# Experts stage: TensorE's loop over the jobs entered twice, the turns of the first rows inside its body

## The chip, the cores and the metric

One Trainium2 chip, one of its cores. The metric is the device time of one execution in microseconds (us), as the median of several runs; lower is better. All matrices are float32; the kernel splits each operand into a high and a low part and takes three products for one.

## The reference, cut to what matters

```python
x = attention(q, k, v)              # 4 x 12 heads, 448 rows, 64 wide, rms-normed q and k
x = x.reshape(1792, 768)            # N tokens, D wide
idx = argmax(norm(x) @ norm(expert_emb).T / tau, axis=1)      # one of 8 experts for a token
for e in range(8):                  # experts
    mask = idx == e
    h = maximum(x[mask] @ w1[e], 0)             # 768 -> 1024
    out[mask] = gate[mask, None] * (h @ w2[e])  # 1024 -> 768
return (sigmoid(out @ w_gate) * (out @ w_val)) @ w_out        # layer 2: 768 -> 1536 -> 768
```

The change is in the second of the three stages, `experts`.

## The kernel before, in words

**Stages.** `attention` (to about 326 us of the profile) computes the tokens' rows, the expert of each and the sorted order; `experts` runs to about 648 us, `layer2` from there to the end. Each engine has an instruction stream of its own; they meet at semaphores. Between two stages is a barrier of all engines.

**Jobs.** The tokens of an expert are taken in jobs of up to T = 294. A job is described by a column of a small table in SBUF, `c.table`, with five rows of J + 1 entries: first token, expert, whether the job is long (more than TS = 256 tokens), column of the list of token numbers, and the number of jobs. VectorE computes it at the start of the stage (`job_table`, L1472 to L1497) and tells by `table_ready`. Each engine reads what it needs from the table into registers of its sequencer with `value_load` (`jobs` at L1286, `long_job` at L1274 and others); in the profile such a load is a TENSOR_LOAD, a FUSED_REGOPS and a SEQ_ASSERT of the helper's line, behind a FUSED_REGOPS for the address when the index is a register. Here there are 8 jobs, 6 short and 2 long.

**One job on TensorE** (`job`, L1592): eight blocks of the first layer (`h`, L1578), each 6 x 3 matmuls, then six blocks of the second (`y`, L1585), each 8 x 3 matmuls, and between the latter the turns (transposes, L1563) of the next job's rows, 6 x 3. Every matmul has a weight load. In the stream the body of a job stands twice, for 256 columns and for 294 (L1625 to L1630): the loop over the jobs (`pe.Fori(0, n_jobs)`) loads `is_long`, and runs the short body or jumps over it (L1627), then jumps over the long body or runs it (L1629), then jumps back (L1625). TensorE's sequencer issues instructions to the array ahead of their execution.

**The start of the stage on TensorE** (L1607 to L1624): 36 idle turns on `tx[0]` (`keep_busy`, L1602), the number of jobs from the table, a wait for cleared banks and for the copied list of tokens, two turns of that list (`tokens_turned`, L1612), six idle turns, a wait for `tokens_out`, and then three times four idle turns and six turns of the first rows (L1621), as each third of the rows has been loaded and scaled by its gates (`gated_dve`, `gated_act`). Then comes the loop.

**The other engines at that point.** GpSimd issues the loads of the first rows (`fetch_rows`, L1110) and then waits in its own loop for turned rows and the first product. ScalarE copies slots of layer 2's weights, scales the second third of the rows (L1436), and takes the high parts of the turned rows (L1422). VectorE, in this order: job table, clearing of banks (L1501), low part of the first weights (`w1_split`, L1457), one slot, wait for `tokens_turned` and copy of the turned list (L1511), scaling of the first third (L1532), `w1_split`, scaling of the last third, two slots, the low parts of the turned rows (L1520), four slots, then its loop (L1548). SP writes the list when it is copied and loads the weights of job 0 once the rows are turned (L1316 to L1319).

**Constants.** GpSimd writes 19 small constants in the fourth step of attention (`constants`, L152), each with a wait for the one before.

Of the kernel before, what the change touches and what calls it, by code (L numbers as in the profile page):

```python
# [145 lines left out]
    return r  # L146


CONSTS = 19


def constants(nc, c, r, pool):  # L152

    done = [0]

    def const(i):
        i.then_inc(r.consts, 1)
        done[0] += 1
        pool.wait_ge(r.consts, done[0])
    exact = dict(allow_small_or_imprecise_dtypes=True)  # L160
    J = MAXJOBS
    const(nc.gpsimd.iota(r.rank[:, :, :], [[0, EARLY], [-1, E]], base=E, channel_multiplier=0, **exact))
    const(nc.gpsimd.iota(r.cap[:, :], [[LINES * CHUNKS, E]], base=0, channel_multiplier=0, **exact))
    const(nc.gpsimd.memset(r.half[:, :], 0.5))
    const(nc.gpsimd.memset(r.ones[:, :], 1.0))
    const(nc.gpsimd.memset(r.tri[:, :], 1.0))
    const(nc.gpsimd.affine_select(out=r.tri[:, :], in_=r.tri[:, :], compare_op=ALU.is_ge, fill=0.0, base=0,
                                  pattern=[[-1, P]], channel_multiplier=1))
    const(nc.gpsimd.memset(c.ones8[:, :], 1.0))
    const(nc.gpsimd.memset(r.mask_e[:, :, :], 1.0))  # L170
    const(nc.gpsimd.memset(r.mask_e[:, :, 0], 0.0))
    const(nc.gpsimd.memset(r.mask_l[:, :, :], 1.0))
    const(nc.gpsimd.memset(r.mask_l[:, :, 0], 0.0))
    const(nc.gpsimd.iota(r.lines[:, :], [[1, ROWS]], base=0, channel_multiplier=0, **exact))
    const(nc.gpsimd.iota(r.slots[:, :], [[1, SLOTS]], base=0, channel_multiplier=0, **exact))
    const(nc.gpsimd.iota(r.token[:, :].rearrange("p (b t) -> p b t", t=NT), [[S, B], [1, NT]], base=0,
                         channel_multiplier=NT, **exact))
    const(nc.gpsimd.iota(c.thr[:, :, :], [[0, E], [T, NT + 3]], base=0, channel_multiplier=0, **exact))
    const(nc.gpsimd.memset(c.thr[:, :, 0], -1.0))
    const(nc.gpsimd.iota(c.jnum[:, :, :], [[1, J + 1], [0, E]], base=0, channel_multiplier=0, **exact))  # L180
    const(nc.gpsimd.iota(c.vals[:, 1, :], [[1, E]], base=0, channel_multiplier=0, **exact))
    const(nc.gpsimd.iota(c.vals[:, 3, :], [[CHUNKS, E]], base=0, channel_multiplier=0, **exact))
    assert done[0] == CONSTS


# [1038 lines left out]
def experts(nc, c, w1, w2, w_l2, w_sums, x_rows, table_of_slots, ids):  # L1224
# [4 lines left out]
    with ExitStack() as ctx:  # L1229
# [17 lines left out]
        index_in = sem("index_in")  # L1247
        dve_table = sem("dve_table")
        table_ready = sem("table_ready")
        tokens_turned = sem("tokens_turned")  # L1250
        tokens_out = sem("tokens_out")
        slots_written = sem("slots_written")
# [21 lines left out]
        def long_job(eng, j):  # L1274
            return eng.value_load(c.table[0:1, bass.ds(j + 2 * (J + 1), 1)], min_val=0, max_val=1)
# [175 lines left out]
        def _(dve):  # L1451
# [20 lines left out]
            def job_table():  # L1472
# [23 lines left out]
                chain(nc.vector.tensor_scalar(c.tablef[:, 2, :], c.tablef[:, 2, :], float(TS), None, ALU.is_gt))  # L1496
                nc.vector.tensor_copy(c.table[:, :], c.tablef[:, :, :].rearrange("p a j -> p (a j)")).then_inc(table_ready, 1)  # L1497

            job_table()
            for bank in hb + yb:  # L1500
                nc.vector.memset(bank[:, TS:T], 0.0).then_inc(banks_set, 1)  # L1501
# [43 lines left out]
                x_out(0, kd, first_banks[kd])  # L1545
            for k in range(3, 7):
                slot_low(k)
            with dve.Fori(0, n_jobs) as j:  # L1548
                job_order(w1_split, w2_split, h_out, scale, x_out, lambda j, d: None, j)

        @block.tensor
        def _(pe):
# [51 lines left out]
                for _ in range(turns):  # L1604
                    nc.tensor.transpose(bank[:, 0:128], c.ident[:, :], c.ident[:, :])

            keep_busy(tx[0], 36)  # L1607
            n_jobs = jobs(pe, pe.wait_ge)
            pe.wait_ge(banks_set, HB + YB)
            pe.wait_ge(tokens_copied, 1)  # L1610
            for part in range(2):
                nc.tensor.transpose(hb[2][0:HALF, part * 128:part * 128 + LINES],  # L1612
                                    c.tokens[0:LINES, part * HALF:(part + 1) * HALF],
                                    c.ident[0:LINES, 0:LINES]).then_inc(tokens_turned, 1)
            keep_busy(hb[0], 6)
            pe.wait_ge(tokens_out, 1)
            for a in range(GATHERS):
                keep_busy(hb[0], 4)
                pe.wait_ge((gated_dve, gated_act)[a % 2], a // 2 + 1)
                for kd in range(KD):  # L1620
                    last = nc.tensor.transpose(first_banks[kd][:, a * R:(a + 1) * R], xr[0:R, a, kd * 128:(kd + 1) * 128],  # L1621
                                               c.ident[0:R, 0:R])
                    if a == GATHERS - 1:
                        last.then_inc(x_turned, 1)  # L1624
            with pe.Fori(0, n_jobs) as j:  # L1625
                is_long = long_job(pe, j)
                with pe.If(is_long < 1):  # L1627
                    job(j, TS)
                with pe.If(is_long > 0):  # L1629
                    job(j, T)  # L1630


def layer2(nc, c, w_l2, w_sums, ids_dram, out):
# [435 lines left out]
def build(nc, q, k, v, g_q, g_k, emb, tau, w1, w2, w_gate, w_val, w_out, out):  # L2069
# [4 lines left out]
    with ExitStack() as ctx:  # L2074
# [12 lines left out]
        with ExitStack() as kept:  # L2087
            def far(name, shape, dt=F32):
                return kept.enter_context(nc.sbuf_tensor(name, shape, dt, side="right"))
            c.table = far("table", [1, 5 * (MAXJOBS + 1)], I32)  # L2090
            c.raw1 = far("raw1", [128, 4, KD, 128])
            c.W1H = far("W1H", [128, 2, KD, 128], F32R)
            c.W1L = far("W1L", [128, 2, KD, 128], F32R)
# [70 lines left out]
```

## Time and profile before

| | |
|---|---|
| Median of 3 runs | 1143.29 us (1142.89 to 1144.02) |
| The profiled execution | 1147.7 us, its span 1146.2 us |
| Mean granted clock of TensorE | 0.986 |
| PE busy | 1110.0 us (97%), 7378 matmuls and turns |
| PEld (weight loads) busy | 983.0 us (86%), 7379 |
| DVE busy | 776.2 us (68%) |
| ACT busy | 600.0 us (52%) |
| POOL busy | 367.7 us (32%) |

Times in the profile are microseconds from the start of the span. PE is TensorE's array, PEld its weight loads; a q behind an engine's name (PEldq) marks an instruction of its sequencer, which keeps no array busy: branches, register operations, loads from SBUF into registers, waits. A group's row reads: line, engine, operation, tiles written and read, shape, count | busy us, mean ns of one | idle us before them, and what ended the idle time; "issue" means that no other engine's signal did. The granted clock is the share of full speed that TensorE had.

### The profile page before, as it was taken

How to read it: one execution, taken by the hardware profiler on the slowest of the kernel's cores; microseconds unless marked ns; L12 is line 12 of the kernel's file. 1: busy time of each engine (PE TensorE's matmuls, PEld its weight loads, DVE VectorE, ACT ScalarE, POOL GpSimd, SP SyncE). 2: the span in 40 equal slices, each digit the busy share in tenths (PEclk: the TensorE clock that was granted, in tenths of full speed). 3: DMA queues.
4: the chain of work that ended last, by engine and by line, in shares of the span. 5: the costliest groups of instructions: out<-in, count | busy, mean ns of one | idle time of the engine just before them, and what ended most of it. 6: DMA issues, size and time to landing. Idle time of an engine off the chain costs nothing. (4 is left out here: it accounts for less than half of the span.)

```text
span 1146.2 us, 22052 instructions
## 1 busy us (share of the span) xinstructions
PE 1110.0 (97%) x7378; PEld 983.0 (86%) x7379; DVE 776.2 (68%) x1411; ACT 600.0 (52%) x1415; POOL 367.7 (32%) x367
## 2 busy tenths in 40 slices
PE   7999999999979899999999899999999999999997
PEld 6666666666679899999999899999999999999997
DVE  5778888897776455665556886475569675574672
ACT  4877877877536455565555653242245343441441
POOL 7797888888531110111011502000003012000002
PEclk9999999999989899999999999999999999999999
DMA  4345564543438666786688342242331334331312
GB/s 125 92 138 164 167 202 144 151 119 109 126 76 210 165 179 172 210 213 187 168 207 220 96 125 83 63 125 63 97 111 42 111 106 151 102 104 49 112 42 97
DMA packets 207778, 149.62 MB, mean 131 GB/s; under 512 B 12446, under 2 KB 203550, under 8 KB 207718
## 3 DMA queue, kind: packets, MB, share of 16 engines
q1 hardware_dynamic: 203446, 133.79, 41.9%
q0 software_dynamic: 3568, 14.82, 4.4%
q8 instruction: 35, 0.57, 0.2%
q10 hardware_dynamic: 704, 0.23, 0.1%
q14 instruction: 25, 0.20, 0.1%
HBM read 128.29 MB, written 20.53 MB: 130 GB/s over the span
## 5 line engine op out<-in xcount | busy, mean ns | idle before, releaser
L2027 PE MATMUL qb<-BH,l_WH 128*128 128x448 f32 x504 | 185.9, 369 | 3.2 <-DVE BL L1897 3.2
L2029 PE MATMUL qb<-BH,l_WL 128*128 128x448 f32 x504 | 185.9, 369 | 0.0
L2028 PE MATMUL qb<-BL,l_WH 128*128 128x448 f32 x504 | 185.9, 369 | 0.0
L1732 ACT ACTIVATE l_WH<-stream 128x384 fp32r<-128x384 f32 x209 | 100.7, 515 | 127.4 <-PE ob L2050 102.4
L1968 POOL TENSOR_TENSOR quads<-quads 128x448 f32<-128x448 f32 x24 | 30.6, 1277 | 381.8 <-DVE quads L1836 381.8
L1836 DVE TENSOR_TENSOR quads<-qb,quads 128x448 f32<-128x448 f32 x168 | 100.2, 621 | 67.5 <-PE qb L2029 67.3
L1832 DVE TENSOR_TENSOR l_WL<-stream,l_WH 128x384 fp32r<-128x384 f32 x209 | 121.5, 600 | 20.4 <-ACT l_WH L1732 20.4
L803 ACT ACTIVATE PR<-sc,negmax 112x448 f32<-112x448 f32 x192 | 120.7, 641 | 15.5 <-DVE negmax L535 14.7
L1573 PE MATMUL hb<-XH,W1H 128*128 128x256 f32 (+1 forms) x384 | 112.6, 293 | 5.3 <-issue 4.3
L1573 PE MATMUL yb<-HH,W2H 128*128 128x256 f32 (+1 forms) x384 | 112.9, 294 | 0.4 <-DVE W2L L1515 0.4
L2048 PE MATMUL ob<-l_WH,GH 128*128 128x384 f32 x336 | 112.5, 335 | 0.4 <-DVE Y L1916 0.4
L2050 PE MATMUL ob<-l_WH,GL 128*128 128x384 f32 x336 | 112.3, 334 | 0.0
L2049 PE MATMUL ob<-l_WL,GH 128*128 128x384 f32 x336 | 112.3, 334 | 0.0
L1575 PE MATMUL hb<-XH,W1L 128*128 128x256 f32 (+1 forms) x384 | 111.5, 290 | 0.0
L1574 PE MATMUL hb<-XL,W1H 128*128 128x256 f32 (+1 forms) x384 | 111.4, 290 | 0.0
L1574 PE MATMUL yb<-HL,W2H 128*128 128x256 f32 (+1 forms) x384 | 109.8, 286 | 0.0
L1575 PE MATMUL yb<-HH,W2L 128*128 128x256 f32 (+1 forms) x384 | 109.7, 286 | 0.0
L535 DVE TENSOR_REDUCE negmax<-sc 112x2 f32<-112x896 f32 x96 | 101.8, 1083 | 10.5 <-PE sc L928 10.4
L2027 PEld LDWEIGHTS qb<-BH,l_WH 128*128 128x128 f32 x504 | 95.1, 189 | 12.6 <-issue 3.3
L2029 PEld LDWEIGHTS qb<-BH,l_WL 128*128 128x128 f32 x504 | 95.1, 189 | 9.2
L2028 PEld LDWEIGHTS qb<-BL,l_WH 128*128 128x128 f32 x504 | 95.0, 189 | 9.1
L1457 DVE TENSOR_TENSOR W1L<-raw,W1H 128x384 fp32r<-128x384 f32 x132 | 68.1, 557 | 50.4 <-ACT W1H L1411 49.0
(259 smaller groups left out, 2552.5 us busy)
## 6 DMA issues: line engine op xcount, KB each, us to landing
raw<-in_moe_w_dram SPq DMA_DIRECT2D x68, 384.0 KB, 5.2
stream<-in_moe_w_dram SPq DMA_DIRECT2D x48, 512.0 KB, 4.7
stream<-w_sums SPq DMA_DIRECT2D x92, 192.0 KB, 2.4
w_sums<-Sb SPq DMA_DIRECT2D x12, 768.0 KB, 6.3
stream<-in_moe_w_out_dram SPq DMA_DIRECT2D x48, 192.0 KB, 2.4
stream<-in_moe_w_val_dram SPq DMA_DIRECT2D x36, 192.0 KB, 2.8
stream<-in_moe_w_gate_dram SPq DMA_DIRECT2D x33, 192.0 KB, 2.6
raw<-in_q_dram SPq DMA_DIRECT2D x24, 224.0 KB, 3.3
```

Source lines behind the costliest of these rows:

```text
L535: nc.vector.tensor_reduce(negmax[:, n % 2, j, :], sc[j % 2][0:P, :, 0:S], AX.X, ALU.max, negate=True).then_inc(maxed, 1)
L803: nc.scalar.activation(PR[:, h, j, :], sc[j % 2][0:P, h, 0:S], ACT.Exp, bias=negmax[:, s, j, h:h + 1], accum_out=den[:, s, h, j:j + 1]).th ...
L1573: nc.tensor.matmul(out[:, 0:n], WH[:, slot, k, :], mh, start=(k == 0), stop=False)
L1574: nc.tensor.matmul(out[:, 0:n], WH[:, slot, k, :], ml, start=False, stop=False)
L1575: last = nc.tensor.matmul(out[:, 0:n], WL[:, slot, k, :], mh, start=False, stop=(k == blocks - 1))
L1832: nc.vector.tensor_tensor(W(c.WL, n), c.stream[:, n % RING, :], W(c.WH, n).bitcast(F32), ALU.subtract).then_inc(c.w_lo, 1)
L2027: nc.tensor.matmul(bank, wh, bh, start=(k == 0), stop=False)
L2028: nc.tensor.matmul(bank, wh, bl, start=False, stop=False)
L2029: mm = nc.tensor.matmul(bank, wl, bh, start=False, stop=(k == 2))
L2048: nc.tensor.matmul(bank, GH[:, f, at], W(c.WH, slot), start=(f == 0), stop=False)
L2049: nc.tensor.matmul(bank, GH[:, f, at], W(c.WL, slot), start=False, stop=False)
L2050: mm = nc.tensor.matmul(bank, GL[:, f, at], W(c.WH, slot), start=False, stop=(f == 3))
```

## The change

TensorE's loop over the jobs becomes a loop with two passes (`entry` 0 and 1) around a loop over jobs. How many jobs a pass has, and the first one's number, come from four integers in SBUF, `c.entries`. For the first pass they are constants, written by GpSimd: first 0, count 1. For the second VectorE computes them from the table: the first job is 1 if job 0 is short and 0 if it is long, the count is the number of jobs less that. VectorE tells by `entries_known`, once before the job table and once before its own loop. The order in the body is turned round: the long body comes first and only in the second pass, then, only in the first pass, the turns of the first rows (`first_turns`, with 8 idle turns instead of 36 at its head), then a second load of `is_long` and the short body. In the first pass the one job is run if it is short; if it is long, that pass runs the turns alone.

```diff
@@ constants
-CONSTS = 19
+CONSTS = 21
+    const(nc.gpsimd.memset(c.entries[:, 0:1], 0))
+    const(nc.gpsimd.memset(c.entries[:, 2:3], 1))
@@ experts, VectorE
+            dve.sem_inc(entries_known, 1)
             job_table()
...
             for k in range(3, 7):
                 slot_low(k)
+            chain(nc.vector.tensor_scalar(c.late[:, 0, 0:1], c.tablef[:, 2, 0:1], -1.0, 1.0, ALU.mult, ALU.add))
+            only(nc.vector.tensor_copy(c.entries[:, 1:2], c.late[:, 0, 0:1]))
+            nc.vector.tensor_tensor(c.entries[:, 3:4], c.tablef[:, 4, 0:1], c.late[:, 0, 0:1], ALU.subtract).then_inc(dve_table, 1)
+            dve.wait_ge(dve_table, n_dve[0] + 1)
+            dve.sem_inc(entries_known, 1)
             with dve.Fori(0, n_jobs) as j:
@@ experts, TensorE
-            keep_busy(tx[0], 36)
-            n_jobs = jobs(pe, pe.wait_ge)
-            pe.wait_ge(banks_set, HB + YB)
-            pe.wait_ge(tokens_copied, 1)
...
-            with pe.Fori(0, n_jobs) as j:
-                is_long = long_job(pe, j)
-                with pe.If(is_long < 1):
-                    job(j, TS)
-                with pe.If(is_long > 0):
-                    job(j, T)
+            def first_turns():
+
+                keep_busy(tx[0], 8)
+                pe.wait_ge(banks_set, HB + YB)
+                pe.wait_ge(tokens_copied, 1)
...
+
+            with pe.Fori(0, 2) as entry:
+                pe.wait_ge(entries_known, entry + 1)
+                first = pe.value_load(c.entries[0:1, bass.ds(entry, 1)], min_val=0, max_val=1)
+                count = pe.value_load(c.entries[0:1, bass.ds(entry + 2, 1)], min_val=1, max_val=J)
+                with pe.Fori(0, count) as k:
+                    j = k + first
+                    with pe.If(entry > 0):
+                        is_long = long_job(pe, j)
+                        with pe.If(is_long > 0):
+                            job(j, T)
+                    with pe.If(entry < 1):
+                        first_turns()
+                        pe.wait_ge(table_ready, 1)
+                    is_long = long_job(pe, j)
+                    with pe.If(is_long < 1):
+                        job(j, TS)
@@ build
+            c.entries = far("entries", [1, 4], I32)
```

What is left out inside `first_turns` is unchanged: the turns of the list of tokens, the idle turns, and the turns of the first rows with their waits.

## Rows read from the trace of the kernel before

**Rows 1.** The page, busy us and share of the span.

```profile
PE 1110.0 (97%) x7378; PEld 983.0 (86%) x7379; DVE 776.2 (68%) x1411; ACT 600.0 (52%) x1415; POOL 367.7 (32%) x367
```

**Rows 2.** Groups by line and shape, TensorE, 338 to 650 us.

```profile
L1573 PE MATMUL hb<-XH,W1H 128*128 128x256 f32 x288 | 83.6, 290 | 5.3 <-issue 4.3 <-DVE XL L1520 0.6 <-DVE W1L L1457 0.4
...
L1563 PE MATMUL tx<-ident,xr 98*128 98x98 f32 x144 | 18.8, 247 | 0.8 <-DVE XL L1520 0.8
```

**Rows 3.** Timeline of TensorE: start, duration in us, what [idle before it].

```profile
380.79 0.58 PE L1573 MATMUL hb<-XH,W1H 128*128 128x256 f32 x1 [4.34 <-issue]
```

**Rows 4.** Line L1629: count, ns min/median/max, first and last start.

```profile
L1629 PEldq COMPARE_BRANCH  x8: 73/210/4879, 374.2 to 645.7; - x8
```

**Rows 5.** DMA queues in 376:378, 382:650, 650:1146 and 369.8:371.8: packets, MB, share.

```profile
q8 instruction: 1, 0.02, 3.0%
...
q1 hardware_dynamic: 84197, 42.76, 60.8%
q0 software_dynamic: 1904, 7.24, 10.4%
...
q8 instruction: 21, 0.34, 0.3%
...
q8 instruction: 1, 0.02, 4.2%
```

**Rows 6.** Windows: us, PE, PEld, DVE, ACT, POOL busy (count), clock, DMA share, GB/s.

```profile
379.25:386.08 6.83, 5.29 (x25) 5.29 (x26) 0.40 (x1) 0.96 (x3) 0.28 (x1) 0.50 0.21 62
386.08:389.50 3.42, 3.42 (x30) 3.42 (x30) 2.24 (x6) 2.05 (x5) 2.25 (x3) 1.00 0.42 123
...
652.30:655.70 3.40, 3.40 (x11) 2.99 (x10) 3.40 (x8) 3.40 (x8) 0.00 (x0) 0.50 0.26 9
```

**Rows 7.** Lines L1625 and L1275, TensorE's sequencer in 494 to 497 us.

```profile
L1625 PEldq ALU_OP  x1: 36/36/36, 494.9 to 494.9; - x1
L1625 PEldq COMPARE_BRANCH  x1: 213/213/213, 495.0 to 495.0; - x1
L1625 PEldq FUSED_REGOPS  x1: 59/59/59, 495.2 to 495.2; - x1
...
L1275 PEldq TENSOR_LOAD <-table x1: 300/300/300, 495.4 to 495.4; - x1
L1275 PEldq FUSED_REGOPS  x1: 151/151/151, 495.7 to 495.7; - x1
L1275 PEldq SEQ_ASSERT  x1: 18/18/18, 495.9 to 495.9; - x1
```

**Rows 8.** Timeline of TensorE: first products of jobs 4 and 2, of layer 2.

```profile
496.74 0.28 PE L1573 MATMUL hb<-XH,W1H 128*128 128x256 f32 x1
...
419.36 0.40 PE L1573 MATMUL hb<-XH,W1H 128*128 128x294 f32 x1
...
651.11 0.44 PE L2027 MATMUL qb<-BH,l_WH 128*128 128x448 f32 x1 [3.16 <-DVE BL L1897]
```

**Rows 9.** Timeline of TensorE and VectorE at the start of the stage.

```profile
327.04 4.13 PE L1605 MATMUL tx<-ident 128*128 128x128 f32 x36 [1.14 <-PEq L192]
...
337.28 0.33 PE L1621 MATMUL tx<-ident,xr 98*128 98x98 f32 x2
...
338.53 0.58 PE L1573 MATMUL hb<-XH,W1H 128*128 128x256 f32 x1 [0.58 <-DVE XL L1520]
...
332.30 0.34 DVE L1511 CAST tokens_T<-hb 84x196 uint32<-84x196 f32 x1
...
335.93 0.62 DVE L1532 TENSOR_SCALAR xr<-xr 98x768 f32<-98x768 f32 x1 [1.33 <-DMA xr<-x_rows,index]
```

**Rows 10.** Line L1587, the sequencer's step before a block of the second layer, 367:370.

```profile
L1587 PEldq ALU_OP  x1: 36/36/36, 368.3 to 368.3; - x1
```

**Rows 11.** Timeline of GpSimd's constants, and of TensorE at 77 us.

```profile
69.61 0.10 POOL L179 MEMSET thr<- 1x8 f32 x1
...
77.31 0.60 PE L911 MATMUL tqk<-ident,qkn 112*128 112x112 f32 x4 [1.92 <-POOL qkn L307]
```

More of the change, by code:

```diff
@@ L1249, in experts @@
         table_ready = sem("table_ready")
+        entries_known = sem("entries_known")
         tokens_turned = sem("tokens_turned")
@@ L1605, in keep_busy @@
                     nc.tensor.transpose(bank[:, 0:128], c.ident[:, :], c.ident[:, :])
-            keep_busy(tx[0], 36)
-            n_jobs = jobs(pe, pe.wait_ge)
-            pe.wait_ge(banks_set, HB + YB)
-            pe.wait_ge(tokens_copied, 1)
[L1611 to L1624, printed above, removed]
@@ L1625, in _ @@
-            with pe.Fori(0, n_jobs) as j:
-                is_long = long_job(pe, j)
-                with pe.If(is_long < 1):
-                    job(j, TS)
-                with pe.If(is_long > 0):
-                    job(j, T)
+            def first_turns():
+                keep_busy(tx[0], 8)
+                pe.wait_ge(banks_set, HB + YB)
+                pe.wait_ge(tokens_copied, 1)
+                for part in range(2):
+                    nc.tensor.transpose(hb[2][0:HALF, part * 128:part * 128 + LINES],
+                                        c.tokens[0:LINES, part * HALF:(part + 1) * HALF],
+                                        c.ident[0:LINES, 0:LINES]).then_inc(tokens_turned, 1)
+                keep_busy(hb[0], 6)
+                pe.wait_ge(tokens_out, 1)
+                for a in range(GATHERS):
+                    keep_busy(hb[0], 4)
+                    pe.wait_ge((gated_dve, gated_act)[a % 2], a // 2 + 1)
+                    for kd in range(KD):
+                        last = nc.tensor.transpose(first_banks[kd][:, a * R:(a + 1) * R], xr[0:R, a, kd * 128:(kd + 1) * 128],
+                                                   c.ident[0:R, 0:R])
+                        if a == GATHERS - 1:
+                            last.then_inc(x_turned, 1)
```

## The prediction

> **What bounds the kernel now.** First the page: TensorE is busy for 1110.0 of 1146.2 us [rows 1]. Time that TensorE alone wins or loses goes straight into the span, wherever nothing else is late. Next, the groups of instructions of the experts' stage [rows 2]: of 5.3 us of idle time before the first layer's matmuls, 4.3 are put down to "issue", so to no other engine. The timeline places them before 380.79, where job 1 begins [rows 3]. The branch rows of TensorE's sequencer explain them: L1629, the test that skips the long body, ran eight times, one of them took 4879 ns where the median is 210, and the first began at 374.2 [rows 4], before the array was done: the sequencer runs ahead of it. In the DMA view a packet of queue 8, "instruction", falls into 376 to 378; from 382 to 650 that queue has none [rows 5]. So the first jump over code not yet fetched waited for it, and then the whole loop was held. The stop costs more than its idle time: the granted clock was 0.50, TensorE's lower level, from 379.25 to 386.08, after TensorE had stood idle; 25 matmuls took 5.29 us, where at 1.00 30 take 3.42 [rows 6]. 25 x 0.12 = 3.0, so 2.3 more. Together 4.3 + 2.3 = **6.6 us**, all that the change can win here.
>
> **Between two jobs.** The sequencer's steps at 495 [rows 7]: add 0.036, branch back 0.213, address 0.059, table load 0.300, bounds 0.151 and 0.018. Ahead of them stands L1629, taken, 0.210; a branch not taken is its shortest, 0.073 [rows 4]; behind them come a branch not taken and three register operations (0.04 to 0.06) for the waits of the first product. From the start of the add (494.9) to that of the last bound (495.9) are 1.0 us for 0.76 of durations: some 0.06 between two steps. In all 11 steps, 1.2 + 0.66 = 1.9 us, begun at 494.6. The next job's first matmul starts at 496.74 with no gap [rows 8]. So the lead is about 2.1 us and 1.9 fit in; after a long job's matmuls (294 columns instead of 256) the same number of instructions is 2.4 us.
> The same prices for the new loop. The jobs are short, short, long, short, short, long, short, short (the first long one starts at 419.36 [rows 8]).
> - Short to short: add, branch back, add for j, branch, load (4 steps), two taken branches (over the long body, over the turns), a second load (4), branch, three register operations: 18 steps, 2.05 + 18 x 0.06 = 3.1 us. Less 2.1, and 0.1 because the weight load isn't ahead either: 1.1 idle, twice.
> - Long to short: branch, load, branch first, then the same: 24 steps, 3.0 + 1.4 = 4.4; less 2.4, plus 0.1: 2.1 idle, twice.
> - Short to long: 1.8, hidden as now, twice.
> - Job 0 to job 1, by the outer loop, two loads of entries more: 30 steps, 3.3 + 1.8 = 5.1; less 2.1, plus 0.1: 3.1 idle, but no fetch: what it jumps to has been there.
> Plain boundaries: 2 x 1.1 + 2 x 2.1 = **+6.4 us**.
> The Trainium skill ("Advanced Engine Details and Errata", Control Flow Timing) gives about 108 ns for a compare-and-branch; that lies between the trace's 0.073 for one not taken and 0.21 for one taken. With its figure for the taken ones the plain boundaries would come to about 4.8, an estimate.
>
> **Clock after the new gaps.** 3.4 us at 0.50 lose 1.5 by [rows 6]. The 3.16 us gap before layer 2 [rows 8] was followed by 0.50 from 652.3 to 655.7 [rows 6]. So for the 3.1 us gap +1.5. For the two of 2.1 no row decides: bounds 0 and 3.0, I take the middle, +1.5. For those of 1.1 I take 0.
>
> **The start.** TensorE now comes to its far jump at once: free at 327.0 (its turns start at 327.04 [rows 9]), two loads of entries at 0.8 each, a few register steps: jump at 329.2. It skips the long body, 647 instructions by the code (288 matmuls and 18 turns, each with a weight load, and 35 waits), which are not there. For the stop I take the one measured, 4.88, bounds 3.8 and 4.9 (the packet came late in a busy DMA then): 334.1. What hides it now: 36 idle turns until 331.17 and the rows' turns after them. The cover is too short in two places.
> First, VectorE waits in order for the tokens' turn. It came before its copy at 332.30 [rows 9]; now it comes at 335.4, the copy at 336, the scaling of the first rows, the weight split and then the scaling of the last rows follow at their old distances (0.74, 0.53, 1.0), the last at about 338 instead of 335.93 [rows 9]. With the slack behind it: **+1.6** at least.
> Second, code comes in packets: 21 for layer 2's 5040 matmuls and weight loads and 187 waits, about 250 instructions each [rows 5]. The one in 369.8 to 371.8 [rows 5] is asked for when the sequencer enters new code, some 2 us before (374.2 to 376.6 at the jump). Around 368.3 it issued L1587 of y(4) [rows 10], by the code 542 instructions into the short body, 702 from the start of TensorE's block, give or take 10. The new jump's target is at 667: some 35 instructions before that edge, and the turns have 93. The next packet is asked for on arrival, and takes 1.5 to 2 to start, 1 to transfer and 1.5 until use: about 4.3, so 338.4. Then some 25 turns of 0.112 (4.13 / 36 [rows 9]) are left before the last rows' turns, 2.8, and 1.25 from those to the first product (337.28 to 338.53 [rows 9]): 342.4 instead of 338.53, **+3.9 us**, high end 5.0. The first product is slow already now (0.58 us long [rows 9]) and will be: 0.
>
> **Small items.** GpSimd gets two memsets in its row of constants, 0.10 each [rows 11] and as much for the wait behind each; the work after them is on the way to the product for which TensorE waits 1.92 us at 77.31 [rows 11]: **+0.4**, bounds 0 and 0.4. VectorE's sem_inc and five small operations before its loop, about 0.7, fall into a wait for ScalarE there; without that cover, 0.7. SP's loads of weights and GpSimd's next gather are issued after the turns and the first product as before, and shift along; no queue is passed. TensorE's short waits for VectorE inside jobs (0.4 and 0.8 us [rows 2] and some as short) shrink, since the others catch up in the new gaps: -1.2.
>
> **Sum**: 3.9 + 0.4 - 6.6 + 3.1 + 1.5 + 6.4 + 1.5 - 1.2 = +9.0 us. The profiled execution took 1147.7 (span 1146.2), 4.4 above the median of 1143.29; taken to the median, **1152.3 us**.
>
> **Rivals.**
> 1. The stop is hidden under the rows' load and the boundaries stay hidden. It decides if the sequencer's lead is over 4.4 us, not 2.1. Then the 6.6 goes and 0.4 comes: 1137.1, faster. Against it: L1629 began at 374.2, and the array ran out at 376.45. Chance 0.09.
> 2. One stop at the start only (the target lies past the edge, or two packets come at once) and no slow clock after the 2.1 us gaps: 1.6 + 0.4 - 6.6 + 3.1 + 1.5 + 6.4 - 1.2 = +5.2, or +3.7 if the clock also holds after the 3.1: 1147.0 to 1148.5. Chance 0.16.
> 3. The steps between jobs cost 1 us less than I count (a load or test merged): gaps 2.1, 1.1, 1.1, 0, 0. With the start of rival 2, 1.6 + 0.4 - 6.6 + 2.1 + 2.2 - 1.2 = -1.5: 1141.8; with mine 1144.1. Chance 0.05.
> 4. The loop, some 120 instructions longer, is no longer held, and jumps fetch again: 6.6 at each of six more boundaries, about 1190. The present loop jumps back over 1300 instructions seven times without a packet [rows 5], so chance 0.02. The Trainium skill ("Runtime: NRT & Kernel Launch", Instruction fetch mechanics) says that a taken branch to outside a window of two blocks must fetch; by that rule this rival would be right, and today's loop would stop seven times, which the trace denies.
> The forecast has 0.68.
>
> **Numbers.** 0.2% (2.3 us) is about what a measurement of this kernel can tell from no change. Faster by more: 0.09 (rival 1); within: 0.06 (rival 3 and a tail of 2); slower: 0.85. The range takes in rival 2, half of 3 and nearly all high ends (5.0 for the start, 3.0 for the clock, gaps a tenth longer): 1144.5 to 1158.
>
> **What would show it.** Right: a compare-branch of TensorE of 4 to 5 us at about 329, a second stop of the array until about 338, the first product near 342; no long branch after that; idle time put down to "issue" of about 3.1 us before job 1 and 2.1, 1.1, 2.1, 1.1 before jobs 3, 4, 6, 7. Wrong: jobs that follow without a gap, or a first product at 338.5.

## The result, and the profile after

The changed kernel takes **1152.2 us** (median of 6 runs, 1149.94 to 1155.64); the kernel before, run beside it, 1143.91 (1142.89 to 1147.10). The ratio is 1.0072, 95% interval 1.0052 to 1.0091: slower by 8.3 us, where 9.0 had been forecast. The profiled execution took 1151.0 us, its span 1149.5.

The spans of the two profiled executions differ by 3.3 us only. Attention was 4.3 us shorter in the one of after: TensorE's block of the stage begins at 322.5 instead of 326.8 (the rows of its first signal, below). The profile of before has three spells of the lower clock in attention, 6.8 us at 24.3, 3.4 us at 78.9 and 6.8 us at 317.8; that of after has only the last of them (6.8 us at 313.4). At 1.5 us for 3.4 us of the lower level [rows 6] the two others make some 4.5 us, an estimate. Such spells come and go from run to run in code that nobody touched. So lengths inside the experts' stage are compared here.

The first signal of TensorE's block by its line, in the kernel before and in the one after:

```profile
L1553 PEldq EVENT_SEMAPHORE  x1: 51/51/51, 326.8 to 326.8; - x1
```

```profile
L1562 PEldq EVENT_SEMAPHORE  x1: 51/51/51, 322.5 to 322.5; - x1
```

**The jump.** The branch over the long body in the first pass, by its line, from 322 to 332 us, is a stop of the forecast size (4.88 had been taken):

```profile
L1642 PEldq COMPARE_BRANCH  x1: 4476/4476/4476, 325.0 to 325.0; - x1
```

No other execution of it in the stage is long (median 0.087 us), and from 370 to 652 us queue 8 has no packet of instructions: the new loop is held too.

**The start**, timeline of TensorE:

```profile
329.64 1.96 PE L1614 MATMUL tx<-ident 128*128 128x128 f32 x8 [8.07 <-issue]
331.40 0.53 PE L1622 MATMUL hb<-ident,tokens 98*84 98x98 f32 x2
331.73 2.31 PE L1614 MATMUL hb<-ident 128*128 128x128 f32 x10
...
335.76 0.33 PE L1631 MATMUL tx<-ident,xr 98*128 98x98 f32 x2
...
337.02 0.38 PE L1582 MATMUL hb<-XH,W1H 128*128 128x256 f32 x1 [0.58 <-DVE XL L1524]
```

VectorE's timeline, copy of the turned list and scaling of the first and last thirds:

```profile
331.97 0.36 DVE L1515 CAST tokens_T<-hb 84x196 uint32<-84x196 f32 x1 [3.92 <-PE hb L1622]
332.93 0.62 DVE L1536 TENSOR_SCALAR xr<-xr 98x768 f32<-98x768 f32 x1 [0.60 <-issue]
...
334.40 0.62 DVE L1536 TENSOR_SCALAR xr<-xr 98x768 f32<-98x768 f32 x1
```

Against [rows 9] the copy comes 9.5 us after the stage's first signal instead of 5.5, the last scaling after 11.9 instead of 9.1, the first product after 14.5 instead of 11.7: **+2.8**. The second stop of the array that I had forecast, until about 338, is not there. What is there: 8 idle turns in 1.96 us, twice as long each as the 36 of [rows 9] (4.13). TensorE had stood idle for 8.07 us and got the lower clock. From 329.64 to the last of the rows' turns it has no idle time: 46 turns in a row, 20 of them at the lower clock. VectorE's last scaling is done at 335.02, and the turns that need it begin only at 335.76. So the array's own row of turns set the first product, and VectorE's late list did not.

The 2.8 compares two single profiles. In the profiles of the five kernels below that start as the kernel before does (the one with two more reads, the one with more constants, the three with its hint) the first product comes 10.8 to 12.5 us after the first signal, so against them the changed start is 2.0 to 3.8 us longer.

**The boundaries.** Timeline of TensorE, the first products of jobs 1, 3, 4, 6 and 7; those of jobs 2 and 5 have no idle time ahead:

```profile
377.33 0.38 PE L1582 MATMUL hb<-XH,W1H 128*128 128x256 f32 x1 [2.89 <-issue]
...
458.03 0.38 PE L1582 MATMUL hb<-XH,W1H 128*128 128x256 f32 x1 [1.89 <-issue]
...
495.30 0.39 PE L1582 MATMUL hb<-XH,W1H 128*128 128x256 f32 x1 [0.85 <-issue]
...
574.92 0.38 PE L1582 MATMUL hb<-XH,W1H 128*128 128x256 f32 x1 [1.89 <-issue]
...
613.58 0.38 PE L1582 MATMUL hb<-XH,W1H 128*128 128x256 f32 x1 [0.86 <-issue]
```

The view's idle time leaves out what the last product's modelled end covers. I count a gap from the start of the last product to the start of the next, less the 0.12 us (0.13 behind a long job) between two products. By that count they are 3.05, 0, 2.06, 1.02, 0, 2.06, 1.03; the 4.34 of [rows 3] is 4.50. Forecast: 3.1, 0, 2.1, 1.1, 0, 2.1, 1.1.

**The clock.** Windows of after (columns as in [rows 6]), the turns at the start and then behind the first, the second and the fourth of these gaps:

```profile
329.60:333.90 4.30, 4.26 (x21) 4.25 (x22) 1.33 (x3) 0.94 (x1) 0.00 (x0) 0.50 0.20 51
```

```profile
378.20:381.60 3.40, 3.40 (x18) 3.40 (x18) 0.11 (x1) 0.67 (x2) 0.00 (x0) 0.51 0.08 25
458.00:461.50 3.50, 3.47 (x29) 3.48 (x30) 0.38 (x1) 0.93 (x3) 0.27 (x1) 1.00 0.41 120
576.20:579.60 3.40, 3.40 (x19) 3.40 (x17) 0.82 (x2) 1.24 (x3) 0.48 (x1) 0.50 0.10 30
```

The lower level (0.50) came behind the gap of 3.05 and behind one of the two of 2.06, and kept off behind the other.

**The stage in sum.** From [rows 3, 8, 9] and the rows above, with job 2's first product at 415.00 and layer 2's at 654.39 in after:

| us | before | after | difference |
|---|---|---|---|
| first signal to first product | 11.7 | 14.5 | +2.8 |
| to job 1's first product | 42.26 | 40.31 | -1.95 |
| to job 2's | 38.57 | 37.67 | -0.90 |
| to layer 2's | 231.75 | 239.39 | +7.64 |

Together +7.6, and layer 2 is as long as before (from there to the end 495.1 in both).

### The profile page after: what moved, and what is told of

The parts are those of the page before. It is cut to its first block and busy times, and to the rows that moved or that the text cites. A ratio compares the mean times of both kernels' runs of the same rounds, so it can differ in the third digit from the quotient of the medians.

```text
span 1149.5 us, 22076 instructions
## 1 busy us (share of the span) xinstructions
PE 1103.5 (96%) x7350; PEld 978.5 (85%) x7351; DVE 769.8 (67%) x1414; ACT 599.6 (52%) x1415; POOL 367.2 (32%) x369
## 5 line engine op out<-in xcount | busy, mean ns | idle before, releaser
L537 DVE TENSOR_REDUCE negmax<-sc 112x2 f32<-112x896 f32 x96 | 101.8, 1082 | 11.7 <-PE sc L930 11.6
```

The source lines that it names most:

```text
L537: nc.vector.tensor_reduce(negmax[:, n % 2, j, :], sc[j % 2][0:P, :, 0:S], AX.X, ALU.max, negate=True).then_inc(maxed, 1)
```

## The experiments

"Gaps" are counted as above, for jobs 1 to 7. "Stage" is the time from TensorE's first signal to the start of the last job's last product: 320.9 us in the kernel before, 328.7 in the changed one. Ratios are against the kernel before on the same chip.

### The jump first, the loop left as it was

```diff
+            with pe.Fori(0, 2) as entry:
+                with pe.If(entry > 0):
-            keep_busy(tx[0], 36)
+                    keep_busy(tx[0], 8)
...
+                    with pe.Fori(0, n_jobs) as j:
```

An empty first pass jumps over the turns and the whole loop and back; the loop has its one read and its order.

> The present loop of before (one table load, short body, then long body) is kept whole; a first, empty pass jumps over the turns and the loop to its end and back, and 8 idle turns stand where 36 did. Theory (the stop at the end of job 0 is a first fetch of the code behind the long body, and what makes the change slow is the sequencer's work at the boundaries, not the jump): one long compare-branch of 4 to 5 us about 0.4 us after the stage begins, none later; job 1 follows job 0 within 0.2 us, no boundary gap above 0.2 us; first product 0 to 2 us later than before, counted from the stage's start; in all 4 to 6.5 us faster than before, about 1138.5. Rival (the sequencer does not hold code that it only jumped to; the hold comes from running through it): the 4 to 5 us at the end of job 0 stays, time as before or up to 2 us slower. Rival 2 (the far jump cannot be hidden; the start pays it): first product 4 us later, time within 2 us of before.

Measured: 1145.14 us, ratio 1.0005 (0.9989 to 1.0021). The empty pass stopped 3.75 us at the start (first product after 12.9 us, +1.1, which is less than what such starts differ by). But the stop at the end of job 0 stayed, as the rival has it. The branch over the long body by its line, and the packets of instructions in 372 to 382:

```profile
L1631 PEldq COMPARE_BRANCH  x8: 73/212/4845, 374.3 to 644.9; - x8
```

```profile
q8 instruction: 3, 0.05, 1.9%
```

What follows: having been jumped to once, early, is not enough. The sequencer then went back and ran the turns and the short body in order, with packets at 341.8, 361.2 and 373.7, and by the time of the branch what lay behind the loop had to be fetched again. All other gaps are 0, so the price of the changed kernel's boundaries isn't in jumps to code that is away.

### Two more reads ahead of the second test

```diff
                 with pe.If(is_long < 1):
                     job(j, TS)
+                is_long = long_job(pe, j)
+                is_long = long_job(pe, j)
                 with pe.If(is_long > 0):
```

> Before, with two more loads of is_long from the table between the short body and the test that skips the long one; nothing else. Theory (the sequencer is about 2.1 us ahead of the array and its 1.9 us of work between jobs just fits; each load with its three register steps is 0.7 to 0.77 us more, all visible): short to short 1.9 + 1.5 - 2.1 + 0.1 = 1.3 to 1.4 us idle, twice more; into a long job one more branch falls through after the loads, 1.3 to 1.6, twice; long to short has no further step, since the loads stand ahead of the long body: none. The stop before job 1 grows by 1.5 or not at all, if the loads run before the stop. In all 6 to 8 us slower, about 1151. Rival (register work hides behind the array): no gaps, time as before.

Measured: 1153.97 us, ratio 1.0075 (1.0047 to 1.0102), gaps 4.87, 2.62, 0.01, 1.04, 2.62, 0.01, 1.11. Between two short jobs stand two reads more, between a short and a long one four, two on either side of the jump back (I had counted that boundary too low), and behind a long one none. The 2.62 less 1.04 are 1.58 us, but not for two reads alone: between the pairs stands the test of the short job, taken here (0.22 us, with 0.06 behind it). The extra reads have no address step either, since the address is already in its register. Their rows, one pair and that branch:

```profile
L1275 PEldq TENSOR_LOAD <-table x2: 297/300/303, 493.4 to 494.1; - x2
L1275 PEldq FUSED_REGOPS  x2: 151/151/151, 493.8 to 494.5; - x2
...
L1627 PEldq COMPARE_BRANCH  x1: 225/225/225, 416.2 to 416.2; - x1
```

From one load to the next are **0.65 us a read**, and 2 x 0.65 + 0.28 = 1.58. With its address step a read in the changed kernel takes 0.82 us (494.06 to 494.88), where 0.77 had been counted from [rows 7]. The expectation of the last run below takes 0.79 from here, which is a read without address and half a branch. The 2.62 before job 5 was followed by the lower clock, that before job 2 by none.

### No idle turns ahead of the list's turns

```diff
-                keep_busy(tx[0], 8)
+                keep_busy(tx[0], 0)
```

> The changed kernel with no idle turns at the head of the first pass (8 in the change). Theory (the start is late because the turns behind the far jump run at the slow clock, 0.213 us each, in order): the tokens' turn comes 8 x 0.21 = 1.7 us earlier and the first product 1.0 to 1.7 us earlier than in the changed kernel; boundaries as there; about 1151. Rival (the second fetch or the rows' scaling sets the start): first product unchanged within 0.3 us.

Measured: 1151.09 us, ratio 1.0054 (1.0031 to 1.0077); the branch stopped 4.63 us, the first product came after 13.9 us instead of 14.5, gaps 3.03, 0, 2.10, 1.00, 0, 2.06, 1.01. The list's turns and VectorE's last scaling both came 1.5 us earlier, but the first product only 0.7: TensorE turned without a break here too (334.48 to 340.3), at the lower level until 338.6, which is 11.6 us after the first signal, where the changed kernel has 11.4. So the level rose no earlier, and what the 8 turns gave back is their time at the full clock, 8 x 0.11 = 0.9, less a stop that was 0.15 longer. That the row of turns sets the first product is shown by this; the 0.7 itself is within what starts differ by. Here the lower clock followed both gaps of 2.1 and not the one of 3.03. So no rule "3.1 brings it, 2.1 half of the time" holds: in the profiles of this kernel, the changed one and the changed one with a hint (below), which have the same gaps, five of nine gaps of 2.0 to 3.1 us were followed by it.

### Long body first, nothing else

```diff
-                with pe.If(is_long < 1):
-                    job(j, TS)
                 with pe.If(is_long > 0):
                     job(j, T)
+                with pe.If(is_long < 1):
+                    job(j, TS)
```

> Before with the two bodies in the other order, long one first, and nothing else. Theory (the stop belongs to the first jump over a body that has not been fetched, wherever it is): a compare-branch of 4 to 5 us right after the rows' turns, first product 3.5 to 4.7 us later than before; no stop before job 1, which follows within 0.2 us; no gaps at the boundaries; time as before within 2 us. Rival (the stop belongs to the loop's first jump back): first product as before, and a stop of 4.3 us before job 1.

Measured: 1148.06 us, ratio 1.0034 (1.0019 to 1.0048): 3.8 us slower by the medians, more than the 2 expected. The profiled execution, 1142.85, was the fastest of ten, and its stage is as long as before's (321.2), so where the 3.8 lie is open. The stop before job 1 is gone, and the first product comes after 15.5 us, +3.8. A stop of 3.4 us stands between the turns and the first product, and a second one where the long body had run for the first time. By their lines:

```profile
L1627 PEldq COMPARE_BRANCH  x8: 77/210/3398, 334.1 to 605.1; - x8
```

```profile
L1629 PEldq COMPARE_BRANCH  x8: 73/76/3824, 337.5 to 605.4; - x8
```

The first line is the jump over the long body; the second is the test of the short one, long once, at 450.5. Timeline of TensorE at job 3, and the packets from 410 to 458:

```profile
456.32 0.38 PE L1573 MATMUL hb<-XH,W1H 128*128 128x256 f32 x1 [3.25 <-issue]
```

```profile
q8 instruction: 5, 0.08, 0.7%
```

What follows: the order alone removes the stop at job 0's end, without a second entry, and puts it ahead of the first product, which comes later by about as much. But five packets came when the long body first ran, and the branch behind it stopped. My reading is that part of that body was not there and that fetching it took the place of what was needed next; the trace shows when packets come, not what they hold.

### The turns in a single loop, and where its jump lands

```diff
+            with pe.Fori(0, n_jobs) as j:
+                is_long = long_job(pe, j)
+                with pe.If(is_long > 0):
+                    job(j, T)
+                with pe.If(j < 1):
             for a in range(GATHERS):
...
+                with pe.If(is_long < 1):
+                    job(j, TS)
```

One read a job, no second entry; sound for this input, whose job 0 is short. Two versions, with 8 and with 36 idle turns at the head, and both with 2 instead of 6 idle turns behind the list's.

> One loop, entered once, with one read of the table as before; its body has the long job first and, behind it, the turns of the rows (passed over from job 1 on) and then the short job. Job 0 jumps over the long body straight to the turns, so that the fetch of code comes while the rows load; this holds for this input alone, where job 0 is short. If my reading is right that a jump leaves the loop held when it lands in the packet that directly follows what was fetched: the stop of 4 to 5 us lies under the rows' load, the first product comes 1 to 2 us later than in the kernel before, no gap at the end of job 0 (-4.5 and -2.3 of slow clock), the boundaries cost 0 to 0.5 us each with one read, and no later stop: -4 to -5 us, ratio 0.996. If a long body passed over once is always fetched again at its first run (as in the run with the long body first), a gap of 3.4 us stands at the end of job 2 and the ratio is 1.000.

> The same kernel with 36 idle turns at its head instead of 8, so that the jump of job 0 lands 56 instructions further on, past the edge of a packet, and one packet of the long body's end is left out by it. If packets are held in the order in which they were fetched, and one left out has to be fetched later, then a stop of 3.5 to 4 us comes at the first run of the long body's end (job 2, so ahead of job 3), with new packets of instructions in the queue there, and the ratio is about 0.3 per cent above that of the same kernel with 8 idle turns. If the place of the edge plays no part, the two kernels have the same gaps. The 28 further idle turns by themselves should cost nothing, as they lie under the rows' load.

Measured with 8: 1144.41 us, ratio 0.9994 (0.9973 to 1.0014), gaps 0.08, 0, 0.26, 0, 0, 0.22, 0.02. Boundaries and hold are as expected. The start is not: the jump came only after the wait for `tokens_out`, at 331.5, took 3.89 us, and the rows' turns were late behind it: first product after 16.9 us, **+5.2** instead of 1 to 2, with the lower clock from 328 to 345. That ate the win.

Measured with 36: 1150.42 us, ratio 1.0053 (1.0038 to 1.0068), gaps 0, 0, **4.20**, 0, 0, 0.26, 0. Branch L1630, the test of the short job, is long once, at 455.5; the packets of instructions in 382 to 650 are five, where the version with 8 has none and no stop:

```profile
L1630 PEldq COMPARE_BRANCH  x8: 65/70/4037, 340.5 to 612.8; - x8
```

```profile
461.80 0.39 PE L1573 MATMUL hb<-XH,W1H 128*128 128x256 f32 x1 [4.02 <-issue]
```

```profile
q8 instruction: 5, 0.08, 0.1%
```

The start differs too: the first jump, the branch L1619, stopped 5.57 us instead of 3.89, the longest such stop of all runs, and the first product came after 18.3 us.

```profile
L1619 PEldq COMPARE_BRANCH  x1: 5567/5567/5567, 332.4 to 332.4; - x1
```

The 28 idle turns ahead of the loop, the only difference in the code, put a stop of 4.2 us at job 3's start, 120 us later. That fits a jump that leaves out a packet, which is then missing, when the code's place against the packets' edges is another; the edges themselves are in no row.

### Twenty more constants

```diff
+    for _ in range(20):
+        const(nc.gpsimd.memset(c.spot[:, :], 0))
```

> The kernel before with twenty more memsets of one element on GpSimd among its constants, each recorded and waited for as the two of the change are. The change's two were priced at 0.2 us each on TensorE's path, because TensorE's wait for the constants at 77 us ends with GpSimd. If so, twenty make that wait 3.6 us longer and everything behind it 3.6 us later: ratio 1.003. If the constants are hidden by other work at the start of the next stage, the time stays, ratio 1.000.

Measured: 1149.23 us, ratio 1.0049 (1.0030 to 1.0067). GpSimd's timeline, the twenty with what follows, and TensorE's wait:

```profile
68.71 2.87 POOL L184 MEMSET spot<- 1x1 int32 x20
71.94 1.04 POOL L450 TENSOR_TENSOR xq<-X 112x512 f32<-112x512 f32 x1 [0.36 <-POOL spot L184]
```

```profile
78.41 0.82 PE L913 MATMUL tqk<-ident,qkn 112*128 112x112 f32 x3 [4.15 <-POOL qkn L309]
```

So the constants do lie on TensorE's path: by the interval 3.4 to 7.7 us for twenty, 0.17 to 0.38 each, though 3.2 us are all that GpSimd needs for them. The wait is 4.15 instead of 1.92 [rows 11], 2.2 us more where 3.6 were expected, and had a spell of 6.8 us at the lower clock behind it, where before had 3.4. For two this gives 0.3 to 0.8. The changed kernel has the two within 0.23 us (68.06 to 68.29); its own wait of TensorE at this place is no longer than before's, so two can't be seen there:

```profile
68.06 0.09 POOL L183 MEMSET entries<- 1x1 int32 x1
68.20 0.09 POOL L184 MEMSET entries<- 1x1 int32 x1
```

```profile
75.12 0.60 PE L913 MATMUL tqk<-ident,qkn 112*128 112x112 f32 x4 [1.86 <-POOL qkn L309]
```

### A hint for the far jump, in the kernel before

```diff
+                if d == 4 and n == TS:
+                    ready = lambda k: k == 2 and hints.append(pe.mark_branch_hint_location())
...
-                with pe.If(is_long > 0):
+                pe.br_lt(is_long, 1, on_true="long_skipped", on_false="long_job").branch_hint(hints[0])
+                with nc.body("long_job", ...):
                     job(j, T)
+                    pe.br("long_skipped")
+                nc.switch_bb("long_skipped")
```

> The loop of the kernel before, with one thing more: inside the short job's body, some 90 instructions ahead of the branch that skips the long job's body, the sequencer is given a hint with that branch's target. Theory 1, the stop of 4 to 5 us at the end of job 0 is nothing but the fetch of code that is asked for only when the branch is reached: asked for about 5 us earlier it lies under the products of job 0. The gap of 4.5 us before job 1 goes to about 0.1, the slow clock that follows it goes too, nothing else moves: about -6.6 us, 1137 us, ratio 0.994. Theory 2, the hint is without effect on a branch this far away: the branch still takes 4 to 5 us, ratio 1.000. Theory 3, the fetch for the hint takes the place of the code that follows the short body in order: a new stop of some 4 us in the last products of job 0 or at the turns, ratio 1.000 to 1.004.

Measured: **1137.46 us, ratio 0.9946 (0.9929 to 0.9962)**, faster than both kernels, and -6.5 us where -6.6 was expected. The hint's line and the branch's (eight executions: the longest takes 0.385 us, where it took 4.88 [rows 4]), and job 1's first product, without idle time:

```profile
L1593 PEldq BRANCH_PREFETCH_HINT  x6: 31/34/55, 366.4 to 632.1; - x6
```

```profile
L1633 PEldq COMPARE_BRANCH  x8: 72/226/385, 371.4 to 636.1; - x8
```

```profile
373.55 0.38 PE L1573 MATMUL hb<-XH,W1H 128*128 128x256 f32 x1
```

No spell of the lower clock follows. Gaps 0, 0.18, 0.01, 0, 0.07, 0.01, 0; stage 313.9. In 382 to 640 three packets of instructions came, while the first long job ran, and nobody waited for them.

Then the same with the hint at other distances (`d == 5`, `k == 1`, and `d == 2`, `k == 2`):

> The loop of before with the hint, but later: in the last block of the short body, some 45 instructions ahead of the branch instead of 90, so about 2.5 us ahead instead of 5. If the fetch takes the same 4.5 to 5 us from the hint on as it did from the branch on, the branch still takes some 2 us, the gap before job 1 is about 2 instead of 4.5, and of the slow clock behind it nothing or 1.5 us stays: ratio 0.996. If a hint needs no such time (or a packet of instructions lands at once when it is asked for), there is no gap and the ratio is 0.994; if a hint so late is lost, the gap is 4.5 and the ratio 1.000.

> The same with the hint earlier: in the third block of the second layer, so ahead of the edge of a packet of instructions that the sequencer passes in the fifth. Theory 1, what was fetched is held as one run in the order of the fetches, and the next packet in order, asked for after the hint, displaces or cuts off what the hint brought: the stop of 4 to 5 us at the end of job 0 is back, ratio 1.000. Rival, a packet once there stays until other code needs its place: no gap, ratio 0.994.

Measured, late: 1138.08 us, ratio 0.9950 (0.9933 to 0.9968). The hint went at 368.18, the branch at 370.14, 2.0 us behind it, and it took 1.58:

```profile
L1633 PEldq COMPARE_BRANCH  x8: 72/226/1577, 370.1 to 635.7; - x8
```

```profile
373.50 0.38 PE L1573 MATMUL hb<-XH,W1H 128*128 128x256 f32 x1 [1.10 <-issue]
```

From the hint the code took 3.5 us to come; a gap of 1.26 was left, and no spell of the lower clock followed. Early: 1137.65 us, ratio 0.9942 (0.9922 to 0.9962), hint at 360.9, 11 us ahead, branch 0.385 us at most, gap 0. The place of the hint is not delicate here: 5 to 11 us ahead serve alike.

The stop that my theory for the early hint expected did not come. But the case that it speaks of did not arise either. The packets of instructions in 360.8 to 372, first with the late hint and then with the early one:

```profile
q8 instruction: 2, 0.03, 1.1%
```

```profile
q8 instruction: 1, 0.02, 0.5%
```

The late hint has a packet at 366.2, some 31 us behind the first product as the kernel before has one at 370.3, and another at 369.3, 1.2 us behind the hint. With the early hint, and with the one 5 us ahead, only one packet stands between the hint and the branch, at 368.2 and 367.5, and it must have brought what the branch jumps to. The early hint's came 7.2 us behind it, so a hint isn't always followed at once. Both of these have three packets during the first long job, and the late one has none from 382 to 640: it seems that the packet in order was left out and fetched then, with nobody waiting. Whether a packet in order can displace what a hint brought stays open.

### The changed kernel with a hint, then with one read

```diff
+            hint = pe.mark_branch_hint_location()
             with pe.Fori(0, 2) as entry:
...
-                    with pe.If(entry > 0):
+                    pe.br_lt(entry, 1, on_true="first_entry", on_false="later_entry").branch_hint(hint)
```

> The changed kernel with the same kind of hint for its own far jump, given as the first thing in TensorE's block, some 2.2 us ahead of the branch. The branch, which took 4.48 us, should take about 2.2 and the idle turns begin 2.2 us earlier; the first product comes about 12.7 us after the start of the stage instead of 14.6, since then the load and the scaling of the rows set it again, as in the kernel before. The boundaries stay: gaps of 3.0, 0, 2.1, 1.0, 0, 2.1, 1.0. So -1.9 us against the changed kernel: 1150.3, ratio 1.0055. If the start's loss does not come from the stop of that branch, the first product stays at 14.6 and the ratio at 1.007.

Measured: 1152.28 us, ratio 1.0070 (1.0047 to 1.0092). In its profile the branch, 2.5 us behind the hint, took 1.64 us instead of 4.48, and the first product came after 12.5 us, 2.1 earlier, as the first theory has it; the gaps are 3.05, 0, 2.05, 1.01, 0, 2.04, 1.03, the stage 326.7, so 2.0 shorter.

```profile
L1643 PEldq COMPARE_BRANCH  x1: 1637/1637/1637, 329.1 to 329.1; - x1
```

The median does not show these 2 us; with intervals of over 2 us to either side it can't refute them either. That the start's loss comes from that stop is shown by the trace, not by the run times.

```diff
+            pe.wait_ge(table_ready, 1)
             with pe.Fori(0, 2) as entry:
...
+                    is_long = long_job(pe, j)
                     pe.br_lt(entry, 1, ...)
...
-                        is_long = long_job(pe, j)
...
-                    is_long = long_job(pe, j)
                     with pe.If(is_long < 1):
```

> The one before with one read of the table less for a job: whether the job is long is read once, ahead of the long body, and the register is used at both tests (TensorE waits for the table ahead of the first pass, which the hint given before it covers). By the price from the run with two more reads, 0.79 us each, the gap before job 1 goes from 3.05 to 2.3, those of 2.06 to 1.3 and those of 1.02 to 0.25: -3.9 us together, and 0 to 1.5 less of slow clock. 1146.3, ratio 1.002. If the boundaries' cost lies in the taken branches and not in the second read, the gaps shrink by less than 0.3 each and the ratio stays where that of the kernel before it in this list is.

Measured: 1149.23 us, ratio 1.0039 (1.0025 to 1.0054), gaps **2.12, 0, 0.41, 0.15, 0, 0.42, 0.15**, in all 5.9 us less than the kernel ahead of it. Groups by shape of TensorE behind the first products, in the one with the hint and in this one:

```profile
L1582 PE MATMUL hb<-XH,W1H 128*128 128x256 f32 x288 | 83.5, 290 | 10.1 <-issue 8.4 <-DVE W1L L1460 0.9 <-DVE XL L1524 0.7
```

```profile
L1582 PE MATMUL hb<-XH,W1H 128*128 128x256 f32 x288 | 82.2, 285 | 4.1 <-issue 2.4 <-DVE W1L L1460 1.0 <-DVE XL L1524 0.6
```

One read is worth 0.86 between two short jobs and 0.93 at the entry; behind a long job two reads went (one behind its body, one for the next), 1.63, which my expectation had as one. The second read, not the taken branches, is what the boundaries cost. But the start was 7 us worse (first product after 19.6): the hint, 6.5 us ahead of the branch with the wait for the table in between, had no effect, and the branch took its full 4.48 us from a later start:

```profile
L1645 PEldq COMPARE_BRANCH  x1: 4479/4479/4479, 332.5 to 332.5; - x1
```

Why this hint was lost, when one 11 us ahead was not, stays open. The wait is one candidate. The packets show another: one came at 327.05, 1.0 us behind the hint, and as the branch still stopped, it was not the one hinted at. In the kernel ahead, the last packet before its hint came at 321.7, 5 us earlier. So here the next packet in order may have been due just when the hint was given; no run separates the two.

## Why the prediction was right, point by point

The total was right, by terms of which most were right and two wrong in opposite directions.

- **What the change can win, -6.6**: right. The gap of 4.5 and its slow clock are what the hint alone returns (-6.5 measured), with nothing else touched.
- **Boundary at the entry, +3.1 and 1.5 of slow clock**: measured 3.05 and one spell of 3.4 us. 30 steps of 0.02 to 0.3 us, read off one boundary of the kernel before and counted, gave it to a tenth.
- **Plain boundaries, +6.4**: 6.17 measured. The lead of 2.1 us, the central assumption (rival 1 needed 4.4), holds at all five gaps. The estimate of 4.8, with the figure of the Trainium skill ("Advanced Engine Details and Errata", Control Flow Timing) for a taken branch, is too low; the taken branches of after are 0.21 like those of before.
- **Clock behind the 2.1 gaps, +1.5**: one of the two, as the middle of the bounds had it; the run without idle turns had both. A draw, not knowledge.
- **The start, +3.9**: the step that failed. The jump and its stop are right (325.0 and 4.48 us for 329.2 and 4.88; the stage began 4.3 earlier). Its second half, "the next packet is asked for on arrival, and takes 1.5 to 2 to start", so a second stop until 338, did not happen: packets came at 326.9, 330.1 and 334.6, the second of them 0.7 us behind the end of the branch instead of 1.5 to 2, and the array never ran out of instructions behind 329.64. In its place stood what I had put at 0: the turns behind the stop ran at the lower clock, 4.2 us for 20 of them, after TensorE had been idle for 8 us, and the 46 turns in a row made +2.8. The floor of +1.6 was too low for another reason: VectorE's last scaling came 2.8 us later, and in the kernel before 0.7 us lay between its end and the turns that need it (336.55 and 337.28), so by VectorE's path alone the start would be 2.1 us later, an estimate.
- **Absorbed waits, -1.2**: wrong. The waits for VectorE at the blocks of the first layer are 1.0 and 0.6 in after where [rows 2] has 0.4 and 0.6. The other engines did not profit from the gaps: VectorE's low part of the weights is late at 342.42 (0.78 us), behind the small operations for the entries, which I had laid under a wait for ScalarE (without it, I had them at 0.7).
- **Constants, +0.4**: within the 0.3 to 0.8 of the run with twenty, but not seen by itself. The lower bound of 0 isn't supported by that run.

By the table above: start +2.8 for 3.9; jobs 0 and 1 together -2.85 for -2.0 (it also holds the loss of a spell at 338.3 that the profiled execution of before had and after had not, 1.5, and the 0.78); the six others +7.6 for 7.9; -1.2 unseen. Start (-1.1) and absorbed waits (+1.2) cancel, and that is luck; what is left, -1.2, is mostly that one spell, and the medians, 8.3 apart, stand between the two sums.

**Rivals.** 1 (all hidden) falls with every gap. 2 (one stop, no slow clock behind the 2.1) had the stop right. Its range of 1147.0 to 1148.5 is too low by a start 1.2 us longer, one spell behind a gap of 2.1 (1.5) and the 1.2 of absorbed waits that did not come. 3 (a step less a boundary) falls. 4 (loop not held) falls: jumps back over 1300 and 1400 instructions ran without a packet. The window of two blocks of which the Trainium skill speaks ("Runtime: NRT & Kernel Launch", Instruction fetch mechanics) does not hold for TensorE here. The same section of the Trainium skill gives TensorE's instruction memory room for 2048 instructions, and that would hold this loop. But the runs show that my confidence, 0.02, came from too simple a picture. Four layouts of nearly the same loop were tried: two held at once, two had one more stop of 3.4 to 4.2 us at job 3. That the changed kernel wasn't one of these I had not worked out; it could have cost 4 to 6 us more.

## What to carry to other kernels

A stop for code that is not there yet shows as one long branch in the sequencer's rows with a packet of instructions beside it; before moving work around to hide it, try a hint on that branch, 5 us ahead: it took 6.5 of the 6.6 us here for one instruction a short job. Count the sequencer's steps between two blocks of work and compare them with its lead over the array: each read of a value from SBUF is 0.65 us here, and 0.8 with the step for its address, and beyond the lead all of it is idle time, every time around. When work moves ahead of a large body of code, or idle turns are added in front of it, look at the branches of the whole loop again, as moving the code by 56 instructions put a stop of 4 us somewhere else.

## What the runs showed of the hardware that I had not expected

- A branch hint takes effect: from hint to code there, 3.5 and 4.1 us (2.0 and 2.5 us ahead of the branch), nothing left to wait for at 5.0 and 11 us ahead. The packet came 1.2 to 1.3 us behind the two given latest and 7.2 us behind the earliest. One, 6.5 us ahead with a wait between and a packet 1.0 us behind it, did nothing.
- Whether a jumped-to stretch stays held depends on what was fetched since, and in what order. One visited early and then left for other code was fetched again (3 packets, 4.85 us); with the jump's target moved by 56 instructions the first run of the long body brought five packets and a stop of 4.0 us instead of none and none.
- A first jump to code that is not there stopped the sequencer for 3.4 to 5.6 us in the ten profiles without a working hint; 3.89 and 5.57 are of kernels that differ by 28 idle turns alone.
- Spells of the lower clock behind gaps of 2 to 3 us come and go: behind one of 3.03 and one of 2.62 there was none, behind others of 2.06 and 2.10 there was. A forecast can only bound them.
